# Two token tiles of twice 480 per batch in place of one of twice 448, with a reordered head

## The chip, the cores and the metric

The kernel runs on one core of one Trainium2 chip. The metric is the device time of one execution in microseconds; the kernel before was timed three times and the median is compared. A profile of one execution stands beside these times. Engines are called PE (TensorE, matmul), PEld (its weight loads), ACT (ScalarE), DVE (VectorE), POOL (GpSimd) and SP (SyncE, which issues most DMAs). PEclk is the TensorE clock that was granted, as a share of its full 2.4 GHz.

## The reference, cut to what matters

```python
B, N, C = 2, 6016, 256            # d_ff = 2048, all float32
qn = q / (norm(q, axis=1) + 1e-6)
kn = k / (norm(k, axis=1) + 1e-6)
s = kn.transpose(0, 2, 1) @ qn / tau          # per batch 256 x 256
a = softmax(s)                                 # over the last axis
x = (v @ a).reshape(B * N, C)
h = x @ w_in                                   # 12032 x 2048
g = maximum(h, 0) + alpha * minimum(h, 0)
return g @ w_out                               # 12032 x 256
```

## The kernel before, in words

**What is multiplied.** For each batch the kernel forms the 256 x 256 scores from 47 blocks of 128 tokens of q and k, takes the softmax, and folds it into the first weight matrix: M = a @ w_in, in eight slices of 256 columns (`make_m`). Then x is never built; each token tile computes v @ M directly. A product in float32 is made of three matmuls in the faster fp32r format: each operand is split into a rounded part (`_hi`) and a remainder (`_lo`), and hi*hi, hi*lo and lo*hi are added up. The ACT makes each hi part by a copy, the DVE each lo part by a subtraction.

**The tiles.** The tokens of a batch are cut into `TILES` = 6 tiles; a tile has two halves of `half_width(T)` tokens: 512 in the first five, 448 in the sixth. For each tile, eight groups G = (T, jp) run, one per slice of 256 hidden units. A group works on 2 x 2 blocks (two blocks of 128 hidden units, two token halves, two halves of the contraction) with a seven-product scheme in place of eight: `up` is called seven times (three matmuls each), on seven mixtures of the v blocks (B11, B22, T1, T3, T2, B21, T4) and seven of M (A11 to S4). The results in the PSUM banks X, Y (named p_ps in the profile) and Z are brought together by ACT (`take_x`) and DVE (`add_part`), `slope` applies the alpha slope, `split_g_hi`/`split_g_lo` split the result, and `down` multiplies it with w_out (four calls of six matmuls) into the four `y_ps` banks. `down` of group G-1 is placed between the `up` calls of group G. So a group has 21 + 24 = 45 matmuls, each as wide as the tile's half, and there are 96 groups.

**The v mixtures.** `load_v` brings the four v blocks of a tile into `v_stage` (SP). For every tile but the first, POOL issues four DMAs that add onto v_stage in place (L423 to L430): T3, T1, T2, and T4; each waits for the lo split of what it overwrites. For the first tile the DVE does these four additions (`mix_first_v`). `split_v_hi` and `split_v_lo` split each mixture, in the order of `V_ACT` and `V_DVE`, one per group.

**The head.** PE runs the 47 score blocks of batch 0 as their loads land (`stage`, tile x_ps in the profile), then `broadcast_rq`, and then fills the time in which the softmax of batch 0 is made with score blocks of batch 1 that were loaded ahead (`late_blocks`, nine of them, `LATE`, a plain float32 product, four matmul records each). In between stand the transposes of the softmax result and the slices 0 and 1 of M (`make_first_m`). Group 0 contains slices 2 and 3 and the last two late blocks. The rest of batch 1's scores are made in pairs of blocks during the tiles 1 to 3 (`pair_blocks`, twelve fp32r matmuls of 256 columns per pair, 19 pairs). The norms and softmax of batch 1 follow in tile 4 (`SOFT_TILE`), its M slices in tile 5 (`M_TILE`) and at the start of tile 6.

**What sets the order.** The program of each engine is written out by hand and runs in that order; semaphores connect the engines. In the head the ACT's order is: raw w_in splits, v splits, root of the norms, table load, `copy_rq`, `exponentials`, `split_at_hi`, the first `split_w_hi`, `take_m`. The w_out pieces that `split_w_hi` needs are loaded by SP (`load_w_out`) after v and the late blocks, on the same DMA queue, and issued when the DVE has added up the squares of batch 0.

Of the kernel before, what the change touches and what calls it, by code (L numbers as in the profile page):

```python
# [5 lines left out]
def build(nc, qk, qk_t, v_t, w_in, w_out, small, y_t):  # L6
# [7 lines left out]
    P = 128  # L14
# [16 lines left out]

    def half_width(T):
        t = T % TILES
        return HALF if t < TILES - 1 else (N - 2 * HALF * (TILES - 1)) // 2

    def first_token(T):
        return T // TILES * N + T % TILES * 2 * HALF
# [7 lines left out]
    B11, B22, T1, T3, T2, B21, T4 = range(7)  # L45
# [9 lines left out]
    LATE = 9  # L55
    LATE_PARTS = (4, 5)
# [22 lines left out]
    with ctx:  # L79
# [88 lines left out]
        m_ps = (*y_ps[0], *y_ps[1])  # L168
# [41 lines left out]
        m_done = sem("m_done")  # L210
# [6 lines left out]
        v_mixed = sem("v_mixed")  # L217
# [45 lines left out]
        W_AT = {1: (6, 7), 2: (8, 9), 3: (10, 11), 4: (12, 13), 6: (14, 15)}  # L263

        V_ACT = {0: (B11,), 1: (B22,), 2: (T1,), 3: (T3,), 4: (T2,), 5: (B21,), 6: (T4,)}
        V_DVE = {0: (B11,), 1: (B22,), 2: (T1,), 3: (T3,), 4: (T2,), 5: (B21,), 6: (T4,)}
        V_ACT_FIRST = {2: (B11,), 3: (B22,), 4: (T1,), 5: (T3, T2), 6: (B21,), 7: (T4,)}
        V_DVE_FIRST = {2: (B11,), 3: (B22,), 4: (T1,), 5: (T3, T2), 6: (B21,), 7: (T4,)}
# [7 lines left out]
        def _(sp):  # L276
# [26 lines left out]
            def load_v(T):  # L303
                b, t = T // TILES, T % TILES
# [4 lines left out]
                n0 = t * 2 * HALF  # L309
# [53 lines left out]
            sp.wait_ge(m_done, JP)  # L363
# [40 lines left out]
        def _(pool):  # L404
# [11 lines left out]
            for T in range(1, ALL):  # L416
                b, t = T // TILES, T % TILES
                H = half_width(T)
                n0 = t * 2 * HALF
# [9 lines left out]
                pool.wait_ge(v_summed[T2], 16 * T)  # L429
# [3 lines left out]
        def _(pe):  # L433
# [56 lines left out]
            def make_m(bank, b, hi, lo):  # L490
                pe.wait_ge(at_hi_ready, b + 1)
                for kc in range(CC):
                    for a_part, parts_of in ((at_hi, (hi, lo)), (at_lo, (hi,))):
                        if a_part is at_lo:
                            pe.wait_ge(at_lo_ready, b + 1)
                        for qc in range(CC):
                            for w_part in parts_of:
                                product = nc.tensor.matmul(  # L498
                                    bank[:, kc * 2 * P:(kc + 1) * 2 * P], a_part[:, qc, kc * P:(kc + 1) * P],
                                    w_part[:, qc, :], start=a_part is at_hi and qc == 0 and w_part is hi,  # L500
                                    stop=a_part is at_lo and qc == CC - 1, skip_group_check=True)
                product.then_inc(m_done, 1)

            def make_first_m(jp):
                fs = slice(jp * 2 * P, (jp + 1) * 2 * P)
                pe.wait_ge(raw_lo_ready, jp + 1)
                make_m(m_ps[jp], 0, w_raw_hi[:, :, fs], w_raw_lo[:, :, fs])
# [10 lines left out]
            def down(G, k):  # L518
# [5 lines left out]
                if jp == 0 and k < 2:  # L524
# [5 lines left out]
                    else:  # L530

                        pe.wait_ge(m_out, CC * (t + 1))
# [45 lines left out]
            late_blocks(5, LATE - 2)  # L578

            for G in range(GROUPS):  # L580
                T, jp = G // JP, G % JP
                if jp == 0:
                    pe.wait_ge(v_lo_ready, NOP * (T + 1))
# [14 lines left out]
                if G == 0:  # L598

                    pe.wait_ge(max_ready, 1)  # L600
# [3 lines left out]
                if G > 0:  # L604
                    pe.wait_ge(c12_done, G)
                else:
                    pe.wait_ge(m_lo_ready, 1)
# [3 lines left out]
                else:  # L611
                    make_first_m(2)
                pe.wait_ge(x_copied, 4 * G + 1)
                up(T, jp, X, S2, T2, False).then_inc(x_done, 1)
# [4 lines left out]
                if G in M_AT:  # L619
                    pe.wait_ge(c11_done, G + 1)  # L620
                    pe.wait_ge(slice_lo_ready, SLICE_AT[G - 1] + 1)
                    make_m(Y, M_AT[G][0], slice_hi, slice_lo)
# [10 lines left out]
                else:  # L633
                    late_blocks(LATE - 2, LATE)
                pe.wait_ge(x_copied, 4 * G + 3)
                up(T, jp, X, A22, T4, False).then_inc(x_done, 1)
# [9 lines left out]
        def _(act):  # L646
            def split_v_hi(T, op):
# [6 lines left out]
                if op in (T1, T3, T2, T4):  # L654
                    if T == 0:
                        act.wait_ge(v_mixed, (T1, T3, T2, T4).index(op) + 1)
                    else:
                        act.wait_ge(v_summed[op], 16 * T)
# [13 lines left out]
            def split_pair_hi(n):  # L672
                act.wait_ge(pair_loaded, 16 * (n + 1))
                if n == 0:

                    act.wait_ge(m_done, JP)
# [15 lines left out]
            def exponentials(b):  # L692
                act.wait_ge(max_ready, b + 1)
                for kc in range(CC):
                    nc.scalar.activation(probs[:, kc, :], scores[:, kc, :], ACT.Exp,
# [12 lines left out]
            def split_slice_hi(n):  # L708
                act.wait_ge(slice_loaded[n % RAW_RING], 16 * (n // RAW_RING + 1))

                act.wait_ge(m_done, M_FIRST + n)
                nc.scalar.copy(slice_hi[:, :, :], w_slice[:, n % RAW_RING, :, :]).then_inc(slice_hi_ready, 1)

            def take_m(b, jp):
                n = JP * b + jp
                mf, bank = (mf0, mf1)[jp % 2], m_ps[jp] if b == 0 and jp < M_FIRST else Y
                act.wait_ge(m_done, n + 1)
# [3 lines left out]
                for kc in range(CC):  # L721
                    part = nc.scalar.mul(mf[:, 2 * kc:2 * kc + 2, :].rearrange("p a f -> p (a f)"),
                                         bank[:, kc * 2 * P:(kc + 1) * 2 * P], row_inv[:, kc:kc + 1])
# [25 lines left out]
            def split_g_hi(G, k):  # L749
# [4 lines left out]
                else:  # L754

                    act.wait_ge(m_done, M_FIRST)
# [25 lines left out]
            load_exp()  # L782
            split_v_hi(0, T1)
            copy_rq(0)
            split_v_hi(0, T3)
            split_v_hi(0, T2)
            exponentials(0)
            split_v_hi(0, B21)
            split_at_hi(0)
            act.wait_ge(sigma_ready, 1)  # L790
            for j in range(3):
                split_w_hi(j)
            split_v_hi(0, T4)
            split_w_hi(3)
# [6 lines left out]
            for j in (4, 5):  # L801
                split_w_hi(j)
            act.wait_ge(m_mixed, 1)
            nc.scalar.copy(m_hi[:, 0, S1:NOP, :], mf0[:, S1 + 1:NOP + 1, :]).then_inc(m_hi_ready, 1)
            take_m(0, 1)

            for G in range(GROUPS):
# [12 lines left out]
                if G == 0:  # L820
                    split_m_hi(0, 1)
                if G == 2:
# [10 lines left out]
                if G == 0:  # L833
                    take_m(0, 2)
# [23 lines left out]
                if G == SUMS_G:  # L858
# [338 lines left out]
```

## Time and profile before

| what | us |
| --- | --- |
| median of 3 runs (lowest, highest) | 1077.02 (1076.87, 1077.05) |
| the profiled execution, as timed | 1076.63 |
| its span from the first to the last instruction | 1074.8 |
| PE busy | 1070.9 |
| DVE busy | 847.0 |
| ACT busy | 654.6 |
| mean granted TensorE clock | 1.000 |

Busy is the time in which an engine has an instruction in work. The matmuls overlap in the records: one that is 512 columns wide is shown as 389 ns long, while the next starts 227 ns later. So the length of one says little here, and the distance between the starts of two neighbours says what a matmul costs. The table's first and second rows differ by 0.4 us; the second is 1.8 us above the span, which is what lies outside the program's instructions.

### The profile page before, as it was taken

To read this page: it belongs to the slowest core of one execution; us is meant where nothing else is said; L and a number is where in the kernel's file an instruction comes from. 1 tells how busy PE (TensorE), PEld (TensorE's weight loads), DVE (VectorE), ACT (ScalarE), POOL (GpSimd) and SP (SyncE) were. 2 spreads that over 40 slices of the span, in tenths; PEclk is the share of its full clock that TensorE was granted. 3 is DMA by queue.
4 is the path that set the end of the run, shared out by engine and by line. 5 is a ranking of instruction groups with operands and counts; after the bars stand their busy time and mean duration, and the time that the engine had idled before them with its cause. 6 is when DMAs were issued, how large, how long until landed. Compare 5 with 4: busy or idle time off the path is not lost.

```text
span 1074.8 us, 13902 instructions
## 1 busy us (share of the span) xinstructions
PE 1070.9 (100%) x4995; PEld 906.2 (84%) x4995; DVE 847.0 (79%) x1349; ACT 654.6 (61%) x1100; POOL 40.4 (4%) x54
## 2 busy tenths in 40 slices
PE   9999999999999999999999999999999999999998
PEld 7888888888888888888998888888888888888898
DVE  6999987877877777787798887777777777787776
ACT  6676677667766555655666655555555555555544
POOL 0000000000000000000000000000000000000000
PEclk9999999999999999999999999999999999999999
DMA  9621154455453102103212101201202202200101
GB/s 382 284 88 50 40 158 127 138 160 150 134 162 99 30 13 54 45 9 79 69 30 73 50 11 49 59 8 52 59 1 59 59 0 54 57 1 10 40 1 35
DMA packets 30837, 80.07 MB, mean 74 GB/s; under 512 B 2992, under 2 KB 9264, under 8 KB 29232
## 3 DMA queue, kind: packets, MB, share of 16 engines
q1 hardware_dynamic: 24288, 67.80, 18.1%
q0 software_dynamic: 6336, 11.28, 6.8%
q8 instruction: 39, 0.64, 0.2%
q14 instruction: 30, 0.25, 0.1%
q10 hardware_dynamic: 144, 0.11, 0.0%
HBM read 64.04 MB, written 12.32 MB: 71 GB/s over the span
## 4 chain that ended last, share of the span: by engine, by line
PE 100%; ACT 0%; issue 0%; POOL 0%; POOLq 0%
PE y_ps L538 47%; PE x_ps L512 24%; PE z_ps L512 12%; PE p_ps L512 6%; PE x_ps L444 4%; PE s_ps L464 3%; PE p_ps L498 2%; PE s_ps L444 1%; PE y_ps L498 1%; PE y_ps L553 0%; PE z_ps L440 0%; PE p_ps L486 0%; PE p_ps L473 0%; PE p_ps L479 0%; ACT y_stage L876 0%; PE s_ps L435 0%
## 5 line engine op out<-in xcount | busy, mean ns | idle before, releaser
L538 PE MATMUL y_ps<-g_hi,w_hi 128*128 128x512 f32 (+1 forms) x760 | 293.1, 386 | 0.0
L538 PE MATMUL y_ps<-g_hi,w_lo 128*128 128x512 f32 (+1 forms) x760 | 292.9, 385 | 0.0
L538 PE MATMUL y_ps<-g_lo,w_hi 128*128 128x512 f32 (+1 forms) x760 | 292.9, 385 | 0.0
L757 ACT CAST g_hi<-h 128x512 fp32r<-128x512 f32 (+1 forms) x384 | 234.0, 610 | 78.6 <-DVE h L1011 69.3
L1011 DVE SCALAR_TENSOR_TENSOR h<-h,small_sb 128x512 f32<-128x512 f32 (+1 forms) x384 | 273.7, 733 | 0.0
L1003 DVE SCALAR_TENSOR_TENSOR h<-z_ps,sigma_neg,h 128x512 f32<-128x512 f32 (+1 forms) x192 | 141.7, 738 | 148.0 <-ACT h L747 147.6
L1045 DVE TENSOR_TENSOR g_lo<-h,g_hi 128x512 fp32r<-128x512 f32 (+1 forms) x384 | 249.9, 670 | 0.8 <-ACT g_hi L757 0.5
L747 ACT ACTIVATE h<-x_ps,sigma_neg 128x512 f32<-128x512 f32 (+1 forms) x192 | 130.7, 681 | 175.2 <-PE x_ps L512 165.1
L747 ACT ACTIVATE h<-x_ps,sigma 128x512 f32<-128x512 f32 (+1 forms) x192 | 130.6, 680 | 124.8 <-PE x_ps L512 120.2
L538 PEld LDWEIGHTS y_ps<-g_hi,w_hi 128*128 128x128 f32 x760 | 142.7, 188 | 27.3 <-issue 0.3
L538 PEld LDWEIGHTS y_ps<-g_hi,w_lo 128*128 128x128 f32 x760 | 142.7, 188 | 27.0
L538 PEld LDWEIGHTS y_ps<-g_lo,w_hi 128*128 128x128 f32 x760 | 142.7, 188 | 26.6
L512 PE MATMUL x_ps<-v_hi,m_hi 128*128 128x512 f32 (+1 forms) x384 | 148.8, 388 | 0.0
L512 PE MATMUL x_ps<-v_lo,m_hi 128*128 128x512 f32 (+1 forms) x384 | 148.1, 386 | 0.0
L512 PE MATMUL x_ps<-v_hi,m_lo 128*128 128x512 f32 (+1 forms) x384 | 148.0, 385 | 0.0
L1003 DVE SCALAR_TENSOR_TENSOR h<-p_ps,sigma,h 128x512 f32<-128x512 f32 (+1 forms) x96 | 70.8, 738 | 42.2 <-ACT h L747 42.2
L512 PEld LDWEIGHTS x_ps<-v_hi,m_hi 128*128 128x128 f32 x384 | 72.1, 188 | 14.4 <-ACT h L747 0.9
L512 PEld LDWEIGHTS x_ps<-v_hi,m_lo 128*128 128x128 f32 x384 | 72.1, 188 | 13.6
L512 PEld LDWEIGHTS x_ps<-v_lo,m_hi 128*128 128x128 f32 x384 | 72.1, 188 | 12.9
L512 PE MATMUL z_ps<-v_hi,m_hi 128*128 128x512 f32 (+1 forms) x192 | 74.3, 387 | 0.0
L512 PE MATMUL z_ps<-v_lo,m_hi 128*128 128x512 f32 (+1 forms) x192 | 74.0, 385 | 0.0
L512 PE MATMUL z_ps<-v_hi,m_lo 128*128 128x512 f32 (+1 forms) x192 | 73.9, 385 | 0.0
(129 smaller groups left out, 1009.4 us busy)
## 6 DMA issues: line engine op xcount, KB each, us to landing
rows_t<-qk_t SPq DMA_DIRECT2D x32, 376.0 KB, 4.0
stage<-qk SPq DMA_DIRECT2D x10, 1024.0 KB, 13.3
v_stage<-v_t SPq DMA_DIRECT2D x20, 512.0 KB, 4.6
y_t<-y_stage SPq DMA_DIRECT2D x20, 512.0 KB, 2.8
pair<-qk SPq DMA_DIRECT2D x19, 512.0 KB, 3.7
v_stage<-v_t POOLq DMA_DIRECT2D x27, 256.0 KB, 4.1
scratch<-w_in SPq DMA_DIRECT2D x12, 256.0 KB, 2.8
v_stage<-v_stage POOLq DMA_DIRECT2D x9, 256.0 KB, 3.3
```

The source lines that it names most:

```text
L444: product = nc.tensor.matmul(s_ps[b][:, kc * C:(kc + 1) * C], rows[:, C + kc * P:C + (kc + 1) * P], rows[:, 0:C], start=False, stop=last, ...
L464: product = nc.tensor.matmul(S[:, kc * C:(kc + 1) * C], k_part[:, i, ks], q_part[:, i, 0:C], start=False, stop=n == PAIRS - 1 and i == 1 a ...
L498: product = nc.tensor.matmul(bank[:, kc * 2 * P:(kc + 1) * 2 * P], a_part[:, qc, kc * P:(kc + 1) * P], w_part[:, qc, :], start=a_part is a ...
L512: product = nc.tensor.matmul(bank[:, 0:H], m_part[:, jp, a, :], v_part[T % 2][:, t, 0:H], start=start and m_part is m_hi and v_part is v_h ...
L538: product = nc.tensor.matmul(y_ps[t][oc][:, 0:H], w_part[:, j, ws], g_part[:, k, 0:H], start=jp == 0 and k < 2 and w_part is w_hi and g_pa ...
L747: nc.scalar.mul(h[:, k, 0:H], X[:, 0:H], side(k)[:, j:j + 1]).then_inc(x_copied, 1)
L757: nc.scalar.copy(g_hi[:, k, 0:H], h[:, k, 0:H]).then_inc(g_hi_ready, 1)
L1003: return nc.vector.scalar_tensor_tensor(out=h[:, k, 0:H], in0=bank[:, 0:H], scalar=side(k)[:, j:j + 1], in1=h[:, k, 0:H], op0=ALU.mult, op ...
L1011: nc.vector.scalar_tensor_tensor(out=h[:, k, 0:H], in0=h[:, k, 0:H], scalar=alpha_sb[:, j:j + 1], in1=h[:, k, 0:H], op0=ALU.mult, op1=ALU. ...
L1045: nc.vector.tensor_tensor(g_lo[:, k, 0:H], h[:, k, 0:H], g_hi[:, k, 0:H].bitcast(fp32), ALU.subtract).then_inc(g_lo_ready, 1)
```

## The change

It does four things.

1. **Widths.** The token tiles of a batch are 512, 512, 512, 512, 480, 480 (twice each) in place of 512 (five times) and 448. The number of tiles, groups and matmuls in them is unchanged, and so is the sum of the columns. Tile 4, with the softmax of batch 1, and tile 5, with its M slices, are now both 480 wide.
2. **Late blocks.** `LATE` is 7 (loaded as 4 and 3) in place of 9, six of them before group 0 and one in it. One pair more (20) is made in the tiles 1 to 3.
3. **The v mixtures.** The first tile gets them from POOL's adding DMAs like all others; the DVE's four additions are gone. In every tile B21 is now split before T2. PE begins group 0 when B21 is split and waits for T2 and T4 on their own.
4. **The order in the head.** On ACT four `split_w_hi` stand before `copy_rq` and three between it and the exponentials; the split of T1 stands between the exponentials and `split_at_hi`. The DVE follows. The maximum and the exponentials are taken per half. The M slices 0 to 3 share the y_ps banks in another way and are handed over by halves. Slice 2 is made before the Z product of group 0. SP issues the second tile's v load after the first two slices. In batch 1, the ACT's table loads stand earlier in their groups.

```diff
+    LEFT = N // 2 - HALF * (TILES - 2)
+    WIDTHS = [HALF] * (TILES - 2) + [LEFT // 2, LEFT - LEFT // 2]
     def half_width(T):
-        t = T % TILES
-        return HALF if t < TILES - 1 else (N - 2 * HALF * (TILES - 1)) // 2
+        return WIDTHS[T % TILES]
...
-    B11, B22, T1, T3, T2, B21, T4 = range(7)
+    B11, B22, T1, T3, B21, T2, T4 = range(7)
...
-    LATE = 9
-    LATE_PARTS = (4, 5)
+    LATE = 7
+    LATE_PARTS = (4, 3)
...
-            load_v(1)
             sp.wait_ge(at_lo_ready, 1)
             for n in range(RAW_RING):
                 load_slice(n)
+            load_v(1)
...
-            for T in range(1, ALL):
+            for T in range(ALL):
...
                 if jp == 0:
-                    pe.wait_ge(v_lo_ready, NOP * (T + 1))
+                    pe.wait_ge(v_lo_ready, NOP * (T + 1) if T > 0 else B21 + 1)
...
                 if G > 0:
                     pe.wait_ge(c12_done, G)
                 else:
+                    make_first_m(2)
                     pe.wait_ge(m_lo_ready, 1)
                 up(T, jp, Z, S1, T1, True).then_inc(z_done, 1)
...
+                if G == 0:
+                    pe.wait_ge(v_lo_ready, T2 + 1)
                 up(T, jp, X, S2, T2, False).then_inc(x_done, 1)
...
-                step(nc.vector.reduce_max(row_max, scores, AX_X))
-                nc.vector.tensor_scalar(neg_max, row_max, -1.0, None, ALU.mult).then_inc(max_ready, 1)
+                for kc in range(CC):
+                    step(nc.vector.reduce_max(row_max[:, kc:kc + 1], scores[:, kc, :], AX_X))
+                    nc.vector.tensor_scalar(neg_max[:, kc:kc + 1], row_max[:, kc:kc + 1], -1.0, None, ALU.mult
+                                            ).then_inc(max_ready, 1)
...
                 dve.wait_ge(x_copied, 4 * G + 1)
+                if G == 1:
+                    split_g_lo(G - 1, 3)
                 add_part(G, Y, 0).then_inc(c11_done, 1)
-                if G > 0:
+                if G > 1:
                     split_g_lo(G - 1, 3)
```

**ACT in the head, from the splits of the raw w_in to the handing over of M's slice 0.** In the names, y_stage holds the loaded w_out, p_ps is the bank of the broadcast and of the transposes, and scratch holds the scores. Before:

```order
L706 CAST w_raw_hi<-w_raw 128x2x256 [waits w_in_loaded] x4
L686 ACTIVATE warm<-ones 128x1
L659 CAST v_hi<-v_stage 128x512 [waits v_mixed]
L690 COPY scratch<-p_ps 128x256 [waits rq_bc_ready]
L659 CAST v_hi<-v_stage 128x512 [waits v_mixed] x2
L695 ACTIVATE scratch,col<-scratch,col 128x256 [waits max_ready]
L695 ACTIVATE scratch,col<-scratch,col 128x256
L659 CAST v_hi<-v_stage 128x512
L701 CAST at_hi<-p_ps 128x512 [waits at_moved]
L664 ACTIVATE w_hi<-y_stage,sigma 128x256 [waits w_out_loaded0,sigma_ready]
L664 ACTIVATE w_hi<-y_stage,sigma 128x256 [waits w_out_loaded0] x2
```

and with the change:

```order
L699 ACTIVATE warm<-ones 128x1
L677 ACTIVATE w_hi<-y_stage,sigma 128x256 [waits w_out_loaded0,sigma_ready]
L677 ACTIVATE w_hi<-y_stage,sigma 128x256 [waits w_out_loaded0] x3
L703 COPY scratch<-p_ps 128x256 [waits rq_bc_ready]
L677 ACTIVATE w_hi<-y_stage,sigma 128x256 [waits w_out_loaded1] x3
L708 ACTIVATE scratch,col<-scratch,col 128x256 [waits max_ready] x2
L672 CAST v_hi<-v_stage 128x512 [waits v_summed2]
L714 CAST at_hi<-p_ps 128x512 [waits at_moved]
L672 CAST v_hi<-v_stage 128x512 [waits v_summed3]
L672 CAST v_hi<-v_stage 128x512
```

The copy of the broadcast (L690, now L703) used to stand ahead of every instruction that needs w_out; now four that wait for the first piece of w_out stand ahead of it.

**DVE in the head, from the scaling of the scores to the lo part of the transposed softmax.** Before:

```order
L960 SCALAR_TENSOR_TENSOR scratch<-x_ps,col,scratch 128x256
L964 TENSOR_REDUCE col<-scratch 128x2 [waits dve_step]
L965 TENSOR_SCALAR col<-col 128x2 [waits dve_step]
L894 TENSOR_TENSOR v_lo<-v_stage,v_hi 128x512 [waits v_hi_ready] x2
L969 TENSOR_SCALAR col<-col 128x2 [waits exp_ready]
L970 RECIPROCAL col<-col 128x2 [waits dve_step]
L894 TENSOR_TENSOR v_lo<-v_stage,v_hi 128x512 [waits v_hi_ready]
L1017 TENSOR_TENSOR at_lo<-p_ps,at_hi 128x512 [waits at_hi_ready]
```

and with the change:

```order
L958 SCALAR_TENSOR_TENSOR scratch<-x_ps,col,scratch 128x256
L963 TENSOR_REDUCE col<-scratch 128x1 [waits dve_step]
L964 TENSOR_SCALAR col<-col 128x1 [waits dve_step]
L963 TENSOR_REDUCE col<-scratch 128x1
L964 TENSOR_SCALAR col<-col 128x1 [waits dve_step]
L915 SCALAR_TENSOR_TENSOR w_lo<-y_stage,sigma,w_hi 128x256 [waits w_hi_ready] x2
L909 TENSOR_TENSOR v_lo<-v_stage,v_hi 128x512 [waits v_hi_ready]
L969 TENSOR_SCALAR col<-col 128x2 [waits exp_ready]
L970 RECIPROCAL col<-col 128x2 [waits dve_step]
L915 SCALAR_TENSOR_TENSOR w_lo<-y_stage,sigma,w_hi 128x256 [waits w_hi_ready]
L1017 TENSOR_TENSOR at_lo<-p_ps,at_hi 128x512 [waits at_hi_ready]
```

The v split that now precedes L969 is that of T1, whose hi part ACT makes only after the exponentials.

## Rows read from the trace of the kernel before

**Rows 1.** The page, parts 1 and 2: busy time, then tenths of 40 slices.
```profile
PE 1070.9 (100%) x4995; PEld 906.2 (84%) x4995; DVE 847.0 (79%) x1349; ACT 654.6 (61%) x1100; POOL 40.4 (4%) x54
...
PEclk9999999999999999999999999999999999999999
```

**Rows 2.** Waits of the weight loads: until 75 us, then from 500 to 600 us.
```profile
PEld x_ps L512 <- ACT h L747: 0.4, 1, 0.4
PEld p_ps L486 <- ACT scratch L695: 0.4, 1, 0.4
PEld z_ps L512 <- DVE m_lo L1094: 0.3, 1, 0.3
...
PEld z_ps L512 <- DVE h L1003: 0.5, 3, 0.2
```

**Rows 3.** PE's timeline (start us, us): first matmul of tiles 8 and 9, 512 wide.
```profile
748.42 0.39 PE L512 MATMUL p_ps<-v_hi,m_hi 128*128 128x512 f32 x1
...
830.02 0.39 PE L512 MATMUL p_ps<-v_hi,m_hi 128*128 128x512 f32 x1
```

**Rows 4.** The same in tile 11, 448 wide: first matmuls of its groups 2 and 7.
```profile
1012.18 0.36 PE L512 MATMUL p_ps<-v_hi,m_hi 128*128 128x448 f32 x1
...
1057.79 0.36 PE L512 MATMUL p_ps<-v_hi,m_hi 128*128 128x448 f32 x1
```

**Rows 5.** PE's timeline: 256 columns, the pair in fp32r, then a float32 stretch.
```profile
154.64 0.28 PE L464 MATMUL s_ps<-pair_hi 128*128 128x256 f32 x1
...
156.07 0.40 PE L512 MATMUL p_ps<-v_hi,m_hi 128*128 128x512 f32 x1
...
41.73 5.35 PE L444 MATMUL x_ps<-stage 128*128 128x256 f32 x24
46.91 0.59 PE L479 MATMUL p_ps<-scratch,ones 128*128 128x256 f32 x2
```

**Rows 6.** PE's timeline in tile 11's first group: six of 512, then 448.
```profile
995.05 0.39 PE L538 MATMUL y_ps<-g_hi,w_hi 128*128 128x512 f32 x1
...
996.44 0.36 PE L512 MATMUL x_ps<-v_hi,m_hi 128*128 128x448 f32 x1
```

**Rows 7.** Stretches: us; busy PE, PEld, DVE, ACT, POOL; PEclk, DMA share, GB/s.
```profile
30.00:38.00 8.00, 8.00 (x38) 7.04 (x38) 7.38 (x7) 6.73 (x8) 0.00 (x0) 1.00 1.02 409
84.65:89.00 4.35, 4.35 (x21) 3.60 (x20) 3.10 (x5) 2.97 (x6) 0.87 (x1) 1.00 0.41 63
109.00:113.30 4.30, 4.30 (x21) 3.53 (x20) 4.07 (x7) 2.65 (x6) 0.86 (x1) 1.00 0.43 61
491.75:493.00 1.25, 1.25 (x8) 1.02 (x6) 1.25 (x3) 0.60 (x2) 0.00 (x0) 1.00 1.01 197
```

**Rows 8.** SP's timeline and the landing times of w_out's first two pieces (min/median/max).
```profile
38.10 0.80 SPq L316 DMA_DIRECT2D y_stage<-w_out  x2
...
DMA to landing us min/median/max: 7.7/8.2/8.6
```

**Rows 9.** ACT's timeline in the head.
```profile
38.98 1.14 ACT L659 CAST v_hi<-v_stage 128x512 fp32r<-128x512 f32 x2 [0.33 <-DMA v_stage<-v_t]
...
47.54 0.37 ACT L690 COPY scratch<-p_ps 128x256 f32<-128x256 f32 x1 [3.19 <-PE p_ps L479]
...
50.68 0.19 ACT L695 ACTIVATION_READ_ACCUMULATOR scratch<-scratch,col 128x1 f32 x1
...
51.62 0.58 ACT L701 CAST at_hi<-p_ps 128x512 fp32r<-128x512 f32 x1 [0.24 <-PE p_ps L486]
52.10 1.31 ACT L664 ACTIVATE w_hi<-y_stage,sigma 128x256 fp32r<-128x256 f32 x3
```

**Rows 10.** DVE's timeline in the head.
```profile
48.85 0.69 DVE L964 TENSOR_REDUCE col<-scratch 128x2 f32<-128x512 f32 x1
...
52.23 0.69 DVE L1017 TENSOR_TENSOR at_lo<-p_ps,at_hi 128x512 fp32r<-128x512 f32 x1
```

**Rows 11.** PE's timeline in the head.
```profile
47.34 3.62 PE L444 MATMUL s_ps<-late 128*128 128x256 f32 x16
50.92 0.66 PE L486 MATMUL p_ps<-ident,scratch 128*128 128x128 f32 x4
...
52.35 0.36 PE L498 MATMUL y_ps<-w_raw_hi,at_hi 128*128 128x256 f32 x1
```

More of the change, by code:

```diff
@@ L167, in build @@
         at_ps = Y[:, :].rearrange("p (c d) -> p c d", c=CC)
-        m_ps = (*y_ps[0], *y_ps[1])
+        m_ps = [[y_ps[jp % 2][kc][:, jp // 2 * C:(jp // 2 + 1) * C] for kc in range(CC)] for jp in range(M_FIRST)]
+        y_halves = [Y[:, kc * C:(kc + 1) * C] for kc in range(CC)]
         zeros_ready = sem("zeros_ready")
@@ L488, in transpose_probs, with make_m @@
                 moved.then_inc(at_moved, 1)
[L490 removed]
+            def make_m(halves, b, hi, lo):
                 pe.wait_ge(at_hi_ready, b + 1)
@@ L715, in take_m @@
                 n = JP * b + jp
-                mf, bank = (mf0, mf1)[jp % 2], m_ps[jp] if b == 0 and jp < M_FIRST else Y
-                act.wait_ge(m_done, n + 1)
+                mf, halves = (mf0, mf1)[jp % 2], m_ps[jp] if b == 0 and jp < M_FIRST else y_halves
+                if n > 0:
+                    act.wait_ge(m_half_done, CC * (n + 1))
                 if n >= 2:
@@ L782, in _ @@
             load_exp()
+            act.wait_ge(sigma_ready, 1)
+            for j in range(4):
+                split_w_hi(j)
+            copy_rq(0)
+            for j in (4, 5, 6):
+                split_w_hi(j)
+            exponentials(0)
             split_v_hi(0, T1)
-            copy_rq(0)
+            split_at_hi(0)
             split_v_hi(0, T3)
-            split_v_hi(0, T2)
-            exponentials(0)
             split_v_hi(0, B21)
[L789 to L794, printed above, removed]
             act.wait_ge(row_inv_ready, 1)
@@ L832, in _ @@
                 take_x(G, 1, 3)
-                if G == 0:
-                    take_m(0, 2)
+                if G == SUMS_G:
+                    nc.scalar.activation(warm[:, :], ones[:, 0:1], ACT.Sqrt)
+                if G == ROOT_G:
+                    load_exp()
                 if G in PAIR_AT:
@@ L857, in _ @@
                     square_rows(n)
-                if G == SUMS_G:
-                    nc.scalar.activation(warm[:, :], ones[:, 0:1], ACT.Sqrt)
-                if G == ROOT_G:
-                    load_exp()
                 if G in SLICE_AT:
@@ L896, in split_v_lo @@
                                         ALU.subtract).then_inc(v_lo_ready, 1)
-            def mix_first_v(what):
-                b11, b12, b21, b22 = (v_stage[:, n, :] for n in range(4))
-                if what == "T1":
-                    dve.wait_ge(v_lo_ready, B11 + 1)
-                    mixed = nc.vector.tensor_tensor(b11, b12, b11, ALU.add)
-                elif what == "T3":
-                    dve.wait_ge(v_mixed, 1)
-                    mixed = nc.vector.tensor_tensor(b12, b22, b12, ALU.add)
-                elif what == "T2":
-                    dve.wait_ge(v_lo_ready, T1 + 1)
-                    mixed = nc.vector.tensor_tensor(b11, b22, b11, ALU.add)
-                else:
-                    dve.wait_ge(v_lo_ready, B21 + 1)
-                    mixed = nc.vector.tensor_tensor(b21, b21, b11, ALU.add)
-                mixed.then_inc(v_mixed, 1)
             def split_w_lo(j):
@@ L1062, in _ @@
             step(nc.vector.reciprocal(tau_inv[:, :], tau_sb))
+            split_v_lo(0, B11)
             for jp in range(M_FIRST):
@@ L1065, in _ @@
             clamp_sums(0)
-            split_v_lo(0, B11)
-            mix_first_v("T1")
             invert_norms(0)
@@ L1070, in _ @@
             split_v_lo(0, B22)
-            mix_first_v("T3")
-            split_v_lo(0, T1)
-            mix_first_v("T2")
+            for j in range(2):
+                split_w_lo(j)
             scale_scores(0)
-            split_v_lo(0, T3)
-            split_v_lo(0, T2)
-            invert_row_sums(0)
-            split_v_lo(0, B21)
-            split_at_lo(0)
-            mix_first_v("T4")
-            dve.wait_ge(sigma_ready, 1)
-            for j in (0, 1):
-                split_w_lo(j)
-            split_v_lo(0, T4)
             for j in (2, 3):
                 split_w_lo(j)
+            split_v_lo(0, T1)
+            invert_row_sums(0)
+            split_w_lo(4)
+            split_at_lo(0)
+            split_v_lo(0, T3)
+            split_v_lo(0, B21)
+            split_w_lo(5)
             combine_m(0, 0)
```

82 lines of the change are left out of this document (44 added, 38 removed).

## The prediction

> **What bounds the kernel now.** I read the page's busy times first: PE is busy for 1070.9 us of a span of 1074.8, with the clock at its full level, 2.4 GHz, in all 40 slices; DVE and ACT have a fifth and more of the span to spare [rows 1]. Then I read what the weight loads waited for: in the first 75 us no wait on another engine's work is over 0.4 us, and in tile 5, where M slices are made, three waits on the DVE add up to 0.5 us [rows 2]. So the time is PE's sum of matmuls plus very little. A change can win or lose in three ways: by the number of columns, by the price of a matmul around its columns, and by letting PE stand still in the head, where its work depends on a chain through ACT and DVE. Last I read the starts of matmuls, because their lengths overlap.
>
> **Part 1, the widths.** The columns of a batch stay the same: 5 x 512 + 448 and 4 x 512 + 2 x 480 are both 3008. So only the price per matmul around the columns can change. Eight groups of tile 8 take 830.02 - 748.42 = 81.60 us [rows 3], which is 10.20 per group and 226.7 ns for each of its 45 matmuls. Five groups of tile 11 take 1057.79 - 1012.18 = 45.61 us [rows 4], 9.12 per group and 202.7 ns per matmul. At 2.4 GHz 512 columns are 213.3 ns and 448 are 186.7, so the surplus is 13.3 ns at 512 and 16.0 ns at 448. Two more widths bear on this [rows 5]. The pair's twelve fp32r matmuls of 256 columns take 1.43 us, 119 ns each, a surplus of about 13. The float32 stretch of 24 records takes 46.91 - 41.73 = 5.18 us, 215.8 ns each; that is 518 cycles for 256 columns, and if a column takes two cycles in float32, the surplus is 2.5 ns. It looks as if a small extra of 2.7 ns is there at most lengths, and is missing for fp32r at 512 and 256 only. And 512 itself loses its low price when it is mixed with 448: six take 996.44 - 995.05 = 1.39 us, 231.7 ns each [rows 6].
>
> No row shows 480. The lower end is the surplus of the neighbour 512: 200 + 13.3 = 213.3 ns, 9.60 per group. The upper end is the surplus of the mixed 512, 18.4: 218.4 ns, 9.83 per group. I take that of 448, the only other width in the trace that is no power of two: 216.0 ns, 9.72 per group. Before, a pair of groups (one 512, one 448) takes 10.20 + 9.12 = 19.32 us; afterwards two of 480 take 19.44. There are 8 such pairs per batch and 2 batches: 16 x 0.12 = **+1.92 us**. The ends give 16 x (19.20 - 19.32) = -1.9 and 16 x (19.66 - 19.32) = +5.4. Half way between the neighbours would be no change.
>
> The Trainium skill (TensorE: Matmul & The Clock Gate, "Wait — 56ns, not 53.3ns?") says that a warm matmul costs its columns plus a fixed 2.5 ns or so, at any width. The float32 row agrees (2.5), the fp32r rows don't (13.3 and 16.0). If the surplus is fixed, as that page has it, 480 costs what the lower end says.
>
> The waits of tile 5 come from the DVE, which has 9.12 us per group there; with 9.7 us they should mostly go: **-0.2 us** of the 0.5 (the records of one wait overlap with the matmul ahead), between 0 and -0.5. Tile 4, with the softmax, gets shorter groups; the DVE's work shrinks with them, and I cost it at nothing.
>
> **Part 2, the late blocks.** Two late blocks are 8 records of 215.8 ns, 1.73 us; the added pair is 1.43 [rows 5]: **-0.3 us** of PE work. ACT and DVE do the pair's splits in their spare time in tile 3. But 1.73 us of filler leave the head, one block of them (0.86 us) ahead of group 0.
>
> **Part 3, the v mixtures by DMA, and the w_out pieces behind them.** POOL issues T3's addition when v has landed, at 38.98 [rows 9], and T1's when B11 is split, at about 40.3 (38.98 + 0.6 for the hi split + 0.7 for the lo split). At that time the late blocks and w_out are being loaded at full rate: 409 GB/s at a DMA share of 1.02 [rows 7]. An addition alone keeps the DMA engines busy for 4.35 x 0.41 = 1.8 us, or 4.30 x 0.43 = 1.8 us, for 256 KB. Where an addition and plain loads meet, the engines are full and only 197 GB/s come through [rows 7], so the two share the same time and neither is free. Two additions are 3.6 us; the two late blocks that are no longer loaded, 524 KB at 409 GB/s, give back 1.3. The first w_out piece was issued at 38.1 and landed 7.7 us later, at 45.8 [rows 8]. It now lands at 45.8 + 3.6 - 1.3 = 48.1 if both additions are served before it; at 46.3 if only T3's is; at 44.5 if neither costs it anything. The additions are issued more than 5 us ahead of that landing and T3's are served in about 4, so I take 48.0.
>
> The Trainium skill (DMA: Bandwidth & Descriptors, "Queues, rings and completion order") says that each DMA engine serves its queues in turn, a packet at a time. By it both additions would be served before w_out is done. The 197 GB/s of the mixed stretch agree.
>
> What waits for w_out is new. ACT now has four `split_w_hi` ahead of `copy_rq`. Three take 1.31 us with 0.40 between starts [rows 9], so four push the copy to 48.0 + 1.65 = 49.65. Before it started at 47.54, as soon as PE had made the broadcast [rows 9]. Until 45.9 the four would be free (they would be done by 47.54); every 0.1 us of a later landing is 0.1 us in the chain copy, scaling, maximum, exponentials, transposes. Queued behind them are `copy_rq` and everything else on ACT; behind the copy the DVE's scaling, and behind that PE's transposes.
>
> **Part 4, the chain itself.** From the copy's start to the last exponential's end it took 50.87 - 47.54 = 3.33 us. The maximum over both halves is 0.69 us [rows 10]; taken by halves, the first exponential starts about 0.3 us earlier, and the second ends about 0.25 earlier. So the chain ends at 49.65 + 3.33 - 0.25 = 52.7. PE's four late blocks last until 47.34 + 16 x 0.216 = 50.8, so it waits 1.9 us, where it waited 0.13 (it began the transposes at 50.92 [rows 11]): **+1.8 us**. What follows moves with it. After the transposes the DVE now does T1's split, the row sums and one w_lo before `at_lo`; that was ready at 52.92 [rows 10] and in the new order comes about 0.3 us later against the transposes (+0.3). Slice 2 ahead of the Z product covers the 0.3 us wait for m_lo (-0.2). Slice 3 alone now covers the ACT's queue in group 0 (+0.2), and the earlier `split_g_lo` in group 1 removes the 0.4 us wait of x_ps [rows 2], worth 0.25 on PE (-0.25). Together **+0.05**; between -0.7, if all that stood still there goes, and +1. Group 0's start (slice 0 of M, now handed over by halves) I expect in time: its chain gains about 0.4 us against `at_lo`, and PE comes 0.5 us after it. T2 and T4 of the first tile are needed some 8 and 12 us after T1's split, and an addition takes about 4.3, the length of its stretch in [rows 7]; no wait.
>
> **The sum.** +1.92 - 0.2 - 0.3 + 1.8 + 0.05 = +3.3 us. The span of 1074.8 becomes 1078.1, the profiled execution's 1076.63 becomes 1079.9. The median of the runs is 0.4 us above the profiled execution; on it I get 1077.02 + 3.3 = **1080.3 us**.
>
> **The rivals.**
> - *480 costs what 512 does (213.3 ns).* For it: the same surplus at 256 and 512. Against it: 448 and the mixed 512. Then part 1 is -1.9 and the sum -0.5: **1076.5 us**. Chance 0.17.
> - *480 lies half way (214.7 ns).* Part 1 is 0: **1078.4 us**. For it only the straight line between the neighbours. Chance 0.09.
> - *The additions don't delay w_out.* If it lands by 45.9, the copy starts at 47.54 as before, and splitting the maximum removes the old wait of 0.13. The head gives -0.1 in place of +1.85: with 216.0 ns **1078.4 us**, chance 0.16. For it: packets of both queues could overlap in time. Against it: the 197 GB/s.
> - *Both: no delay and 213.3 ns.* **1074.5 us**, faster. The other side needs both at once: even with 213.3 ns, from a landing of w_out later than about 46.3 it is within 0.2%. Chance 0.08.
> - *More is lost.* 480 at 218.4 ns gives 1080.3 + 3.5 = 1083.8. Or PE's clock falls to the lower level, 1.2 GHz, after 1.9 us of standing still; no row shows such a pause, and each us of work at that level would add 1 us. From **1082.5 us** on; chance 0.08.
>
> That the widths are not what the text says can be excluded: the sizes are constants. That the head isn't sped up is my forecast.
>
> **How the numbers follow.** The forecast (216.0 ns, w_out at about 48) has the rest, 0.42: 1079.3 to 1081.3. The range leaves out the "both" case and most of "more is lost": 1075.8 to 1082.5. A measurement of this kernel can tell about 0.2%, 2.15 us, from no change. Slower by more than that (over 1079.2) are the forecast (nearly all of it, 0.39) and "more is lost": 0.47. Faster (under 1074.9) is most of "both", and a little for the unforeseen: 0.09. The rest, 0.44, lies between.
>
> **What would show it.** Starts in a tile 480 wide: groups 9.72 us apart (216.0 ns), not 9.60 or 9.66. Landing of the first w_out piece: 48, not 44.5 to 46. ACT's copy of the broadcast at 49.6, with ACT waiting for a DMA ahead of its first w_hi, and PE's transposes at 52.7 behind a wait of 1.9 us. The clock stays at 1.00. The waits in tile 5 shrink. The forecast is wrong if the copy starts by 47.6, or if the groups are below 9.65 us.

## The result and the profile after

| what | before | after |
| --- | --- | --- |
| median of 19 runs each (lowest, highest) | 1076.58 (1076.00, 1077.05) | 1078.77 (1078.32, 1079.49) |
| ratio, with its 95% interval | 1 | 1.0020 (1.0013 to 1.0026) |
| the profiled execution, as timed | 1076.63 | 1079.33 |
| its span | 1074.8 | 1077.5 |
| PE starts the broadcast (end of batch 0's score blocks) | 46.91 | 47.22 |
| from the broadcast to the start of tile 4 | 370.07 | 370.52 |
| from the start of tile 4 to the end of PE's last matmul | 654.97 | 656.83 |

The change makes the kernel slower by 2.2 us. The last three rows split the 2.6 us by which PE's end is later in the profiles. The first 0.31 belongs to no part of the change: up to the broadcast PE's program is the same in both kernels, and over the profiles of this study its start lies anywhere between 46.18 (experiment 2, which has the head of before) and 47.22. Some of the first score matmuls start 0.43 us apart, twice the later 0.216, and how many do so differs from profile to profile; the granted clock of these stretches reads 1.00 in all of them. So I count from the broadcast: the head gives +0.45, all behind tile 3 gives +1.86.

The page of after, busy times and clock; it answers to [rows 1]:

```profile
PE 1073.2 (100%) x4999; PEld 906.9 (84%) x4999; DVE 846.7 (79%) x1350; ACT 655.4 (61%) x1101; POOL 43.8 (4%) x58
...
PEclk9999999999999999999999999999999999999999
```

PE is busy 2.3 us longer (it was 1070.9), with the clock at its full level as before. PE's timeline of after at the start of tile 10, and of groups 0 and 7 of tile 11, all 480 wide; it answers to [rows 4]:

```profile
912.87 0.38 PE L524 MATMUL p_ps<-v_hi,m_hi 128*128 128x480 f32 x1
...
991.21 0.37 PE L524 MATMUL p_ps<-v_hi,m_hi 128*128 128x480 f32 x1
...
1059.45 0.38 PE L524 MATMUL p_ps<-v_hi,m_hi 128*128 128x480 f32 x1
```

Seven groups take 1059.45 - 991.21 = 68.24 us, which is 9.75 each and 216.6 ns per matmul. I had forecast 9.72 and 216.0.

The waits of the weight loads in after, in the first 75 us and then from 75 to 100 us (columns as in [rows 2]: us in total, times, longest):

```profile
PEld x_ps L524 <- ACT h L764: 0.6, 2, 0.3
PEld y_ps L507 <- DVE at_lo L1017: 0.5, 1, 0.5
PEld z_ps L524 <- DVE h L1003: 0.3, 1, 0.3
...
PEld x_ps L524 <- ACT h L764: 0.4, 1, 0.4
```

No wait before the transposes, where I had expected 1.9 us. From 75 to 100 us before has no wait on another engine; the one of after stands in group 2. From 500 to 600 us the list of after is empty, where before had three waits on the DVE [rows 2].

The head of after: ACT's, then PE's, then the DVE's timeline (start us, us; in brackets the idle time ahead and what ended it), answering to [rows 9], [rows 11] and [rows 10]:

```profile
45.30 1.70 ACT L677 ACTIVATE w_hi<-y_stage,sigma 128x256 fp32r<-128x256 f32 x4 [0.46 <-DMA y_stage<-w_out]
47.85 0.37 ACT L703 COPY scratch<-p_ps 128x256 f32<-128x256 f32 x1 [0.84 <-PE p_ps L488]
48.12 1.30 ACT L677 ACTIVATE w_hi<-y_stage,sigma 128x256 fp32r<-128x256 f32 x3
```

```profile
47.65 3.62 PE L453 MATMUL s_ps<-late 128*128 128x256 f32 x16
51.10 0.60 PE L495 MATMUL p_ps<-ident,scratch 128*128 128x128 f32 x4
...
53.47 0.51 PE L507 MATMUL y_ps<-w_raw_hi,at_lo 128*128 128x256 f32 x2 [0.30 <-DVE at_lo L1017]
```

```profile
52.35 0.46 DVE L915 SCALAR_TENSOR_TENSOR w_lo<-y_stage,sigma,w_hi 128x256 fp32r<-128x256 f32 x1
52.73 0.68 DVE L1017 TENSOR_TENSOR at_lo<-p_ps,at_hi 128x512 fp32r<-128x512 f32 x1
```

ACT did wait for w_out, but only 0.46 us, and its four splits were done when PE finished the broadcast: the copy started as early as PE let it. The transposes start 51.10 - 47.65 = 3.45 us behind the late blocks' start, which is 16 times 0.216: no gap.

Why w_out came in time is in the DMA rows: the stretches of after (columns as in [rows 7]), the first adding DMA on POOL, the landing times of all twelve of T3's additions, and those of the first two w_out pieces:

```profile
41.00:43.50 2.50, 2.50 (x17) 2.32 (x16) 2.23 (x6) 0.37 (x2) 0.78 (x1) 1.00 0.99 397
43.50:44.00 0.50, 0.50 (x4) 0.42 (x4) 0.40 (x4) 0.50 (x1) 0.00 (x0) 1.00 1.13 352
44.00:46.50 2.50, 2.50 (x13) 2.22 (x12) 2.28 (x8) 2.03 (x5) 0.00 (x0) 1.00 1.09 210
```

```profile
39.48 1.01 POOL L432 DMA_DIRECT2D v_stage<-v_t  x1 [36.62 <-DMA v_stage<-v_t]
```

```profile
L432 POOL DMA_DIRECT2D v_stage<-v_t x12: 862/862/1011, 39.5 to 902.4; - x12
...
DMA to landing us min/median/max: 3.9/4.2/7.3
```

```profile
DMA to landing us min/median/max: 6.9/8.0/9.1
```

T3's addition is issued at 39.48, but until 43.5 the engines still move plain loads at 397 GB/s, the rate they had without it (409 in [rows 7]). Only then does the rate fall to 210. The addition landed 7.3 us after its issue, where the median is 4.2. The w_out pieces, issued at 38.29 and 38.66, landed 6.9 and 9.1 us later, at 45.2 and 47.8.

### The profile page after: what moved, and what is told of

The parts are those of the page before. It is cut to its first block, busy times and chain, and to the rows that moved or that the text cites. A ratio compares the mean times of both kernels' runs of the same rounds, so it can differ in the third digit from the quotient of the medians.

```text
span 1077.5 us, 13920 instructions
## 1 busy us (share of the span) xinstructions
PE 1073.2 (100%) x4999; PEld 906.9 (84%) x4999; DVE 846.7 (79%) x1350; ACT 655.4 (61%) x1101; POOL 43.8 (4%) x58
## 4 chain that ended last, share of the span: by engine, by line
PE 99%; DVE 0%; ACT 0%; issue 0%; POOL 0%; POOLq 0%
PE y_ps L550 47%; PE x_ps L524 24%; PE z_ps L524 12%; PE p_ps L524 6%; PE x_ps L453 4%; PE s_ps L473 3%; PE p_ps L507 2%; PE y_ps L507 1%; PE y_ps L565 0%; PE z_ps L449 0%; PE s_ps L453 0%; ACT scratch L708 0%; PE p_ps L482 0%; DVE scratch L958 0%; PE p_ps L488 0%; DVE v_lo L909 0%
```

## The experiments

Each edit is against the kernel after, but for experiment 2. All times stand beside runs of the kernel before on the same chip.

**1. The widths undone.** Everything else of the change stays.

```diff
-    WIDTHS = [HALF] * (TILES - 2) + [LEFT // 2, LEFT - LEFT // 2]
+    WIDTHS = [HALF] * (TILES - 1) + [LEFT - HALF]
```

> The changed kernel with the old widths (five tiles of twice 512, one of twice 448), all else as changed. Theory A (the widths are the loss): the trace of the changed kernel has its 32 groups of 480 at 9.75 us, where pairs of 512 and 448 cost 19.32; that is 32 x 0.09 = 2.9 us, of which about 0.5 comes back as the DVE waits in the M groups of tile 5 that 448 had. So about 2.4 us below the changed kernel: 1076.4, no measurable difference from the kernel before (ratio 0.9990 to 1.0005). Theory B (the reordered head is the loss and the widths are neutral): 1078.8, ratio 1.002.

Measured: 1076.71 us (11 runs) beside 1076.76 for before, ratio 1.0000 (0.9991 to 1.0009). From the broadcast to tile 4 it takes 370.45 us, within 0.1 of after; from tile 4 to the end 655.25, against 656.83. So the loss goes with the widths. What the reordered head with its seven late blocks is worth can't be told from the medians (the interval is 0.9 us to either side); up to tile 4 the profile has 0.4 us more than before (370.07), as in after.

**2. The widths alone**, in the kernel before.

```diff
-        t = T % TILES
-        return HALF if t < TILES - 1 else (N - 2 * HALF * (TILES - 1)) // 2
+        return WIDTHS[T % TILES]      # WIDTHS = [HALF] * (TILES - 2) + [480, 480]
...
```

The first token of each tile follows from the same list.

> The kernel before with the new widths alone (four tiles of twice 512, two of twice 480), old head and order. Theory A: groups of 480 at 9.75 us, +2.9 us, less the 0.5 of the waits in tile 5: 1079.0, ratio 1.0022. Theory B: ratio 1.000.

Measured: 1078.22 us (11 runs), ratio 1.0016 (1.0007 to 1.0025), which is +1.7 us with an interval of 0.8 to 2.7; counted from the broadcast, the profile is 2.2 us longer than before's (1025.04 to 1027.25). With experiment 1, where undoing the widths takes 2.1 us off the median, the widths cost 1.5 to 2.2 us and the rest nothing that the medians can tell from 0. One wait separates its tile 4 from that of after. Its third group runs from 436.14 to 446.21, 10.07 us; in after the same group takes 9.76. The weight loads of this kernel between 430 and 450 us, and ACT ahead of them:

```profile
PEld x_ps L516 <- ACT h L751: 0.6, 2, 0.3
```

```profile
437.30 1.28 ACT L863 ACT_TABLE_LOAD   x1
438.60 0.20 ACT L863 ACTIVATE warm<-ones 128x1 f32<-128x1 f32 x1
438.70 0.65 ACT L751 ACTIVATE h<-x_ps,sigma 128x480 f32<-128x480 f32 x1
```

Here the copy of x_ps, which PE waits for, stands right behind the table load. Before shows the same group at 10.48 against 10.20, and two such waits (0.5 together). After and experiment 1 have none; in after this table load starts at 432.60, ahead of another copy of x_ps, and PE doesn't wait for that one. So the last words of part 4 of the change ("the ACT's table loads stand earlier") are worth 0.3 us, which I had not costed. No run moves the table load alone; that it is the cause is read from these rows.

**3. Other widths**, to see what a matmul costs as a function of its columns.

```diff
+    WIDTHS = [508, 504, 500, 496, 488, 512]
```

> The changed kernel with six widths per batch: 508, 504, 500, 496, 488, 512 (same sum). It measures the price of a matmul by width. Theory A (fp32r at a width other than 512 or 256 pays about 3 ns more than 512 does): plain groups of 488 at 45 x (203.3 + 16.7) = 9.90 us, of 496 at 10.05, of 508 at 10.28, which is more than the 10.20 of 512; the kernel at about 1086. Rival 1 (surplus fixed at 13.3 for widths that end on 16 columns or more, 480 being special): 496 at 9.90. Rival 2 (the surplus changes smoothly with the width): 508 below 10.20.

Measured in one run: 1085.60 us, a span of 1083.8. PE's timeline at group 5 of tile 6 (508 wide), groups 0 and 1 of tile 7 and the start of tiles 8 and 9:

```profile
641.08 0.39 PE L524 MATMUL p_ps<-v_hi,m_hi 128*128 128x508 f32 x1
...
671.80 0.39 PE L524 MATMUL p_ps<-v_hi,m_hi 128*128 128x504 f32 x1
...
682.06 0.39 PE L524 MATMUL p_ps<-v_hi,m_hi 128*128 128x504 f32 x1
...
753.47 0.39 PE L524 MATMUL p_ps<-v_hi,m_hi 128*128 128x500 f32 x1
...
833.97 0.38 PE L524 MATMUL p_ps<-v_hi,m_hi 128*128 128x496 f32 x1
```

Seven groups 504 wide take 753.47 - 682.06 = 71.41 us, 10.20 each: as much as at 512. The last three groups 508 wide take 671.80 - 641.08 = 30.72 us, 10.24 each, which is more than at either neighbour. The groups inside the tiles, away from a change of width, give (480 from after, 448 from [rows 4], 512 from [rows 3]):

| columns | us per group | ns per matmul | ns above columns / 2.4 |
| --- | --- | --- | --- |
| 512 | 10.20 | 226.7 | 13.3 |
| 508 | 10.24 | 227.6 | 15.9 |
| 504 | 10.20 | 226.7 | 16.7 |
| 500 | 10.05 | 223.3 | 15.0 |
| 496 | 10.05 | 223.3 | 16.7 |
| 488 | 9.90 | 220.0 | 16.7 |
| 480 | 9.75 | 216.7 | 16.7 |
| 448 | 9.12 | 202.7 | 16.0 |

From 480 to 504 it is a staircase: one step is 8 columns and 3.33 ns, and 500 costs what 496 does. 508 doesn't fit (by the staircase it would cost what 504 does; it costs 0.9 ns more), and 448 lies 0.6 ns below it, so this is no full rule of the cost. 512 costs no more than 504, and that is most of the reason why a width of 512 is worth keeping. 32 groups at 9.75 against 16 pairs at 10.20 + 9.12 = 19.32 are 16 x 0.18 = +2.9 us.

**4. The w_out pieces issued later**, so that they stand behind T3's addition in time.

```diff
+            sp.wait_ge(v_lo_ready, B11 + 1)
             load_w_out(0)
```

> The changed kernel with the two w_out loads of the head issued only after the lo split of B11, about 40.8 us in place of 38.3, so after POOL's first addition (39.5) and about with its second (40.9). Theory C (the DMA engines serve what was issued first, whichever queue): the first addition now goes ahead of w_out, which lands at 46.5 to 48; ACT's copy of the broadcast starts 1 to 2 us later than 47.85, PE waits as long before its transposes, and the time rises by 1 to 2 us. Theory D (plain loads go ahead of the additions in any case): w_out lands by 46.0, the copy is late by 0.2 at most, no difference in time.

Measured: 1079.62 us (6 runs), ratio 1.0030 (1.0019 to 1.0041), some 0.9 us over after. SP's issue of w_out, the first addition, one stretch, ACT and PE (timelines and windows of this kernel):

```profile
40.27 0.87 SPq L325 DMA_DIRECT2D y_stage<-w_out  x2
```

```profile
39.08 1.01 POOL L433 DMA_DIRECT2D v_stage<-v_t  x1 [36.22 <-DMA v_stage<-v_t]
```

```profile
41.00:42.50 1.50, 1.50 (x9) 1.34 (x8) 1.50 (x3) 0.00 (x0) 0.38 (x1) 1.00 1.09 253
```

```profile
46.06 1.71 ACT L678 ACTIVATE w_hi<-y_stage,sigma 128x256 fp32r<-128x256 f32 x4 [1.63 <-DMA y_stage<-w_out]
47.67 0.35 ACT L704 COPY scratch<-p_ps 128x256 f32<-128x256 f32 x1
48.78 1.30 ACT L678 ACTIVATE w_hi<-y_stage,sigma 128x256 fp32r<-128x256 f32 x3 [0.76 <-DMA y_stage<-w_out]
```

```profile
51.12 0.66 PE L496 MATMUL p_ps<-ident,scratch 128*128 128x128 f32 x4 [0.87 <-ACT scratch L709]
```

Here the addition was issued 1.2 us ahead of w_out, and the low rate of an addition (253 GB/s) comes at 41.0 to 42.5; in after, with w_out issued first, it came from 44.0 on. The addition landed 5.4 us after its issue, at 44.5, and w_out's first piece at 46.0; in after w_out's came first, at 45.2, and the addition at 46.8. So between these two the order of issue decided. It is no rule for all: the second part of the late blocks was issued at 25.4 and landed only at 43.2, when the slow stretch had long begun. The price of a late w_out is as part 3 had it: ACT's four splits, then the copy, then PE waits before the transposes. ACT also waits 0.76 us for the second piece, which part 3 never looked at; in after that piece landed at 47.8, 0.3 us before ACT came to it. PE's end is 1.1 us later against its broadcast than in after.

**5. The wait for at_lo.** Besides the widths of experiment 1, `at_lo` is made before one w_lo.

```diff
             invert_row_sums(0)
-            split_w_lo(4)
             split_at_lo(0)
+            split_w_lo(4)
```

> The changed kernel with the old widths, and the DVE's split_at_lo ahead of its fifth split_w_lo in the head. In the changed kernel PE waits 0.46 us for at_lo in slice 0 of M. If that wait is the cost of the new DVE order, it falls by about 0.4 (one w_lo, 0.40 between starts) and the kernel is 0.4 us below e1 (1076.71): 1076.3. Rival: T1's split, one ahead of it, sets at_lo anyway, or group 0 waits as much more: 1076.7.

Measured: 1076.46 us (11 runs), ratio 0.9998 (0.9989 to 1.0007). PE's timeline at the first matmul that reads at_lo:

```profile
52.26 0.28 PE L507 MATMUL y_ps<-w_raw_lo,at_hi 128*128 128x256 f32 x1
52.46 0.50 PE L507 MATMUL y_ps<-w_raw_hi,at_lo 128*128 128x256 f32 x2
```

The two stand 0.20 us apart, where after had 0.57 (52.90 to 53.47). The wait is gone and the profile from the broadcast to tile 1 is 0.37 us shorter than in experiment 1 (96.45 to 96.08), as the DVE's rows above suggest. The medians differ by less than their interval.

**6. And the split of T4 later on ACT**, behind the `take_x` that PE waits for in group 0.

```diff
-                    split_v_hi(0, T4)
...
                 take_x(G, 1, 3)
+                if G == 0:
+                    split_v_hi(0, T4)
```

> e5, and in group 0 ACT's split of T4 behind take_x(0, 1) in place of ahead of it. In the changed kernel PE waits 0.3 us before the S3 product for take_x, behind which the split stands. Expected: that wait falls by 0.2 to 0.3, T4's lo part is still made in time (the DVE is busy with M until then): 1076.0 to 1076.1, ratio to before 0.9993. Rival: T4's lo part comes later and the wait moves to the A22 product: 1076.3.

Measured: 1076.22 us (11 runs), ratio 0.9993 (0.9985 to 1.0002), the lowest median of the study; the interval includes 1, so I claim no version better than before. The wait for ACT in group 0 of this kernel:

```profile
PEld x_ps L524 <- ACT h L764: 0.5, 1, 0.5
```

Two waits of together 0.6 became one of 0.5, and group 0 takes 9.19 us in place of 9.43: a part of the delay only moved to the next place where ACT hands over.

**7. Nine late blocks** with the new head (and the widths of experiment 1).

```diff
-    LATE = 7
-    LATE_PARTS = (4, 3)
+    LATE = 9
+    LATE_PARTS = (4, 5)
```

> The changed kernel with the old widths and nine late blocks again (loaded as 4 and 5, eight of them ahead of group 0). Two late blocks are 1.73 us of PE and the pair that goes is 1.43: +0.3. Their 512 KB are loaded ahead of w_out, 1.3 us: w_out's first piece lands at about 46.5 and its second at 49, the three w_hi ahead of the exponentials end at 50.4, and PE waits about 0.6 us before the transposes: +0.6. Together 1077.6. If w_out's landing doesn't matter: 1077.0. If the larger filler covers waits that the seven blocks leave open: 1076.5.

Measured: 1079.49 us (9 runs), ratio 1.0026 (1.0016 to 1.0035): 2.8 us over experiment 1, three times what I expected. ACT and PE, and two stretches:

```profile
47.17 1.71 ACT L677 ACTIVATE w_hi<-y_stage,sigma 128x256 fp32r<-128x256 f32 x4 [2.78 <-DMA y_stage<-w_out]
48.78 0.35 ACT L703 COPY scratch<-p_ps 128x256 f32<-128x256 f32 x1
```

```profile
51.88 0.66 PE L495 MATMUL p_ps<-ident,scratch 128*128 128x128 f32 x4 [1.58 <-ACT scratch L708]
```

```profile
41.00:42.50 1.50, 1.50 (x10) 1.34 (x9) 1.50 (x4) 0.00 (x0) 0.33 (x1) 1.00 0.97 407
44.00:46.50 2.50, 2.50 (x14) 2.19 (x13) 1.24 (x4) 0.37 (x2) 0.00 (x0) 1.00 1.09 303
```

This is the forecast's picture of the head almost to the number: the copy starts 2.53 us behind the broadcast at 46.25 (forecast 49.65 - 46.91 = 2.74), and PE stands still for 1.6 us before the transposes (its weight load for 2.0). Its cause is that the first piece of w_out lands at 47.1, behind 524 KB more of late blocks (1.3 us). But those explain only 1.3 of the 1.9 us by which it lands later than in after, though it was issued earlier (37.81, not 38.29); from 44.0 to 46.5 the rate is 303 GB/s, between that of plain loads and that of additions, so the w_out pieces shared the engines with additions that were issued 1.2 us after them. So the order of issue alone doesn't tell when an addition is served, and what else does is open. LATE = 7 is what keeps the new head from losing some 2 us.

Three of the nine executions (1080.14, 1080.27 and 1080.32 us) had a mean granted clock of 0.998; the other six (median 1079.33) had 1.000, and so did every other execution of this study. The profiled one is among the six, so where in the three the clock fell is not recorded. Only this kernel has a pause so long in its head, which would fit, but that the pause brought it about is not shown.

**8. The short tile in tile 3** (with the edits of 5 and 6), away from the M slices.

```diff
+    WIDTHS = [HALF] * 3 + [LEFT - HALF] + [HALF] * 2
```

> e6 with the narrow tile of twice 448 moved from place 5, where batch 1's M slices are made, to place 3. In e6's trace (and in the kernel before) six M groups of the 448 tile lose 0.6 us in all to waits for the DVE; a tile of 512 doesn't (0.03 per group). Theory (the DVE is short of time only where a narrow group also makes M): these 0.6 us go, the added border between widths in batch 1 costs 0.1 to 0.2: 0.4 below e6, 1075.8, ratio to before 0.9990. Rival (the waits come from the M slices themselves, or the pairs in tile 3 are now short of time): 1076.2 or more.

Measured: 1076.78 us (11 runs), ratio 1.0002 (0.9993 to 1.0011); a miss by 1 us. The waits of the weight loads of this kernel from 320 to 412 us:

```profile
PEld z_ps L524 <- DVE h L1004: 0.7, 3, 0.2
```

Between 488 and 584 us, in tile 5, its list is empty: the waits for the DVE are gone from there. But tile 3 makes score pairs, and 448-wide groups with a pair wait for the DVE just like 448-wide groups with an M slice. The wait follows the short groups.

## Why the prediction went as it did

The time fell in the range, 1.5 us under the forecast of 1080.3 and next to two rivals of 1078.4. Of the 1.5, 0.4 is that before's median over 19 runs is 1076.58 and not 1077.02; the change itself is +2.2 in place of +3.3. That it fell so near is in part luck. Counted in the profiles from the broadcast, the term for w_out, +1.8, came out at -0.2, and two terms that I had too small made up for most of that: the widths by 1.0 and the head's chain by 0.85. Nearest to what happened is the rival in which the additions don't delay w_out; its 1078.4 also holds a width term and a head (-0.1) that were both too small. The mechanisms came out as follows.

- **Part 1, widths: sign right, size too small.** Forecast +1.92, measured +2.9 for the matmuls alone. The mis-sized term is the surplus of 480: I took the 16.0 ns of the neighbour 448, and it is 16.7. 0.67 ns is little, but it is multiplied by 32 x 45 matmuls. The rivals of 213.3 and 214.7 ns are excluded by 9.75 us per group, and experiments 1 and 2 show the loss with and without the rest of the change. My reading that an extra is missing "for fp32r at 512 and 256 only" holds in so far that none of the six other widths that were run has a surplus under 15.0.
- **The waits of tile 5: right, and more.** Forecast -0.2. Groups of M in before take 10.63 to 10.73 us where 9.12 + 1.43 = 10.55 would be the work, 0.64 over six groups; in after the six take 11.19 or 11.20, where 9.75 + 1.43 = 11.18 is the work, 0.11 over. That is -0.53, at my lower end. My reason to discount it (the records of a wait overlap with the matmul ahead) was wrong for this place.
- **Tile 4 cost at nothing: wrong by 0.3.** In after two waits of PE behind the table load of the batch 1 softmax are gone. I had described the move in the change and not looked at what waited there. Sum of these three: 2.88 - 0.53 - 0.28 = +2.07; the profiles show +1.86 behind the start of tile 4. By batch: from tile 10 to PE's end, where neither wait stands, after takes 161.70 us against 160.33, +1.37 for 8 x 0.18 = 1.44; tiles 4 to 6 take 250.33 against 249.84, +0.49 for 1.44 - 0.81 = 0.63. So some 0.1 us per batch is left, the size by which single groups at a change of width are off their sum.
- **Part 2, late blocks: right.** Eight matmuls of 216 ns go, a pair of 1.43 us comes. From the broadcast to tile 1 after is 1.01 us shorter than before (97.53 to 96.52), of which 1.73 are the blocks; so 0.7 of new waiting stands in the head. With the pair the head comes to 1.43 - 1.01 = +0.42, which is the +0.45 of the table above.
- **Part 3, w_out: the step that failed.** That both additions "are served before it" was the wrong choice between the bounds 44.5 and 48.1. The first piece landed at 45.2, 0.7 above the lower bound, of which 0.2 are its later issue; the rate fell to that of additions only after 43.5. I had argued from the 197 GB/s of a mixed stretch; that shows what the engines deliver once they serve both, and nothing about when they begin to. The second piece did suffer: it lands 1.8 us later than 47.09 - 1.3 + 0.2 (before's landing, less the late blocks, plus the later issue), but still before ACT needed it. My sign that the forecast is wrong ("if the copy starts by 47.6") was set in absolute time: the copy started at 47.85, but both before and after that is 0.63 us behind the start of the broadcast, so in substance the sign was given. The rest of the step held: experiments 4 and 7 show PE standing still for 0.9 and 1.6 us when w_out's first piece comes at 46.0 or 47.1, and the chain from the copy to the last exponential took 50.91 - 47.85 = 3.06 us, where I had 3.08.
- **Part 4, the chain: inside its bounds, near the upper one.** Forecast +0.05 (bounds -0.7 and +1), measured +0.9: the 0.7 of new waiting, and 0.2 that were gained ahead of slice 0 of M. at_lo costs 0.38 us (slices 0 and 1 take 3.50 in place of 3.12), where I had said 0.3. The wait of x_ps in group 1 went as forecast (-0.25: the group takes 10.24 in place of 10.49). What I had wrong is what I put at nothing: group 0 takes 9.43 in place of 9.81 although 0.86 of late block left it, 0.5 of new standing still in three waits; and group 2 has a new wait for ACT and takes 11.90 in place of 11.66. The wait for at_lo is removable (experiment 5), that of group 0 in part (experiment 6).

The Trainium skill (DMA: Bandwidth & Descriptors, "Queues, rings and completion order") has each engine serve its queues in turn, a packet at a time. By it the additions would have begun within the backlog. The windows of after (397 GB/s until 43.5) speak against that; those of experiment 4 (253 GB/s from 41.0, before the late blocks had landed) and of experiment 7 (303 GB/s) speak for it in part. What makes the difference is open: experiment 4 differs in whether w_out is queued ahead of the addition, experiment 7 in 524 KB of late blocks, and no run here looked at the queues' depth alone.

The Trainium skill (TensorE: Matmul & The Clock Gate, "Wait — 56ns, not 53.3ns?") has a fixed 2.5 ns per matmul. For fp32r the eight widths above say 13.3 to 16.7; a cost fixed over all widths is excluded by 504 and 512, which take the same time.

## What to carry to other kernels

Before a tile width is changed, measure the distance between starts at that very width: here 504 and 512 columns cost the same, and 480 twice is 0.9% dearer than 512 and 448. Even tiles do level the load of a helper engine (0.5 us of waits went), but a few tenths of a microsecond of waits don't pay for 2 ns on each of 1440 matmuls. Where a load is to be in time for an in-order engine, issue it ahead of the slower transfers (experiment 4), and look at how much is queued ahead of it (experiment 7). And list the waits of the groups behind the place that was changed as well: one of the new waits here stood at 80 us, behind the stretch that I had looked at.

## What the runs showed of the hardware

- The fp32r matmul of N columns costs N/2.4 plus 16.7 ns at the four multiples of 8 from 480 to 504 (500 costs the same as 496), 15.9 at 508, and 13.3 at 512; so 508 is dearer than both its neighbours. Next to a change of width the 512 loses its low price: the border groups 512 to 480 take 10.09 us where 24 x 226.7 + 21 x 216.7 = 9.99 is the sum.
- After a pause of PE of 1.6 us the granted clock stayed at 1.00 in the profile of experiment 7, in the windows around it and over the whole span. But three of that kernel's nine executions show a mean of 0.998 and took 0.9 us more than the other six. So the rival in which the clock falls after such a pause is not excluded; in after there was no such pause.
- An adding DMA of 256 KB lands after 4.2 us alone and after 7.3 to 8.6 us behind a backlog of plain loads (T3's and T1's additions in after and experiment 7).
